# One core: the bias stage and the attention put into one program, with the first splits spread over four steps

## What is computed

```
scores = q @ k.T / 8
x      = log1p(|i - j|) / log1p(max(i, 1))          # 576 x 576
bias   = relu(x * w1 + b1) @ w2                      # 32 hidden, 8 heads
attn   = softmax(scores + bias);   o = attn @ v
h = o @ w_in;   g = s * relu(h)**2 + b;   x1 = g @ w_out
h = x1 @ w2_in; g = h - tanh(h);          out = g @ w2_out
```

## Time and profile before

| | |
|---|---|
| median of 3 runs | 1180.36 us (1180.12 to 1181.59) |
| the profiled execution | 1182.0 us, of which 1180.2 us is the span of the trace |
| PE busy | 1123.6 us (95% of the span) |
| ACT, DVE, POOL busy | 720.2, 629.5, 597.8 us |
| chain that ended last | PE 85% of the span |

### The profile page before, as it was taken

How to read it: one execution, slowest core, us unless ns; L and a number is a source line. 1 busy time by engine, 2 the same in 40 slices (tenths; PEclk the granted TensorE clock), 3 DMA queues, 4 the chain that set the end, 5 groups by cost and what they waited for, 6 DMA issues and landing times.

```text
span 1180.2 us, 17800 instructions
## 1 busy us (share of the span) xinstructions
PE 1123.6 (95%) x6306; PEld 995.0 (84%) x6306; DVE 629.5 (53%) x1090; ACT 720.2 (61%) x1362; POOL 597.8 (51%) x505
## 2 busy tenths in 40 slices
PE   4659878999999999999999999999999999999998
PEld 1138767999999999999999999999988888999998
DVE  5857775744675366447654754566344063260440
ACT  8957785755676477557665765676455264473552
POOL 1014545566465545655655555555455455555553
PEclk9879998999999999999999999999999999999999
DMA  3577773455445544554455454453233333433332
GB/s 127 209 249 200 217 211 93 151 172 178 139 155 159 175 152 142 163 157 141 162 167 171 138 160 156 149 162 125 81 115 107 107 101 105 131 109 124 97 111 75
DMA packets 69657, 172.47 MB, mean 146 GB/s; under 512 B 8704, under 2 KB 15680, under 8 KB 69568
## 3 DMA queue, kind: packets, MB, share of 16 engines
q1 hardware_dynamic: 69280, 171.24, 46.3%
q10 hardware_dynamic: 288, 0.07, 0.0%
HBM read 155.59 MB, written 15.69 MB: 145 GB/s over the span
## 4 chain that ended last, share of the span: by engine, by line
PE 85%; ACT 1%; issue 0%; DVE 0%; ACTq 0%
PE ps_f L652 23%; PE ps_f L654 23%; PE ps_f L653 23%; PE ps_t L477 6%; PE ps_o L442 3%; PE ps_o L444 3%; PE ps_s L464 3%; PE ps_s L465 3%; PE ps_s L458 0%; ACT p_t L499 0%; ACT pth L490 0%; DVE ptl L556 0%; ACT wh L602 0%; DVE xl L628 0%; DVE p_t L544 0%
## 5 line engine op out<-in xcount | busy, mean ns | idle before, releaser
L609 POOL TENSOR_TENSOR wl<-w_raw,wh 128x512 fp32r<-128x512 f32 x320 | 418.3, 1313 | 441.5 <-ACT wh L602 441.3
L652 PE MATMUL ps_f<-xh,wh 128*128 128x464 f32 (+1 forms) x640 | 239.4, 374 | 5.0 <-issue 5.0
L652 PE MATMUL ps_f<-gh,wh 128*128 128x464 f32 (+1 forms) x640 | 238.8, 373 | 0.0
L654 PE MATMUL ps_f<-xh,wl 128*128 128x464 f32 (+1 forms) x640 | 238.5, 373 | 0.0
L653 PE MATMUL ps_f<-xl,wh 128*128 128x464 f32 (+1 forms) x640 | 238.1, 372 | 0.0
L654 PE MATMUL ps_f<-gh,wl 128*128 128x464 f32 (+1 forms) x640 | 237.4, 371 | 0.0
L653 PE MATMUL ps_f<-gl,wh 128*128 128x464 f32 (+1 forms) x640 | 237.3, 371 | 0.0
L602 ACT ACTIVATE wh<-w_raw 128x512 fp32r<-128x512 f32 x320 | 198.0, 623 | 40.0 <-PE ps_f L654 39.8
L544 DVE CUSTOM_DVE_ANT_0 p_t<-ps_s,bias_t 128x576 f32<-128x576 f32 x160 | 120.0, 750 | 94.0 <-PE ps_s L465 93.3
L675 ACT ACTIVATE r_buf<-ps_f 128x464 f32<-128x464 f32 (+1 forms) x160 | 89.2, 557 | 115.0 <-PE ps_f L654 115.0
L490 ACT ACTIVATE pth<-ps_t 128x576 fp32r<-128x576 f32 (+1 forms) x140 | 91.0, 650 | 91.9 <-PE ps_t L477 89.7
(11 more groups left out here) (74 smaller groups left out, 1536.6 us busy)
## 6 DMA issues: line engine op xcount, KB each, us to landing
w_raw<-in_w_in SPq DMA_DIRECT2D x80, 512.0 KB, 3.8
w_raw<-in_w_out SPq DMA_DIRECT2D x80, 512.0 KB, 3.7
bias_t<-bias_flat SPq DMA_DIRECT2D x128, 288.0 KB, 2.9
bias_flat<-stage SPq DMA_DIRECT2D x36, 295.5 KB, 2.1
q_raw<-in_qt SPq DMA_DIRECT2D x32, 288.0 KB, 3.9
k_raw<-in_kt SPq DMA_DIRECT2D x32, 288.0 KB, 4.5
v_raw<-in_vt SPq DMA_DIRECT2D x32, 160.0 KB, 4.1
bias_t<-bias_flat SPq DMA_DIRECT2D x32, 144.0 KB, 4.1
```

The lines of the kernel that those rows point to most:

```text
L609: pool.tensor_tensor(wl[:, b % RING, :, :], w_raw[:, b // 2 % RAW, b % 2, :, :], wh[:, b % RING, :, :].bitcast(F32), ALU.subtract).then_in ...
L652: pe.matmul(acc, hi, rhs_h[:, k0 + kk, 0:T], start=(first and kk == 0), stop=False)
L654: mm = pe.matmul(acc, lo, rhs_h[:, k0 + kk, 0:T], start=False, stop=(last and kk == 3))
```

## The change

- One block in place of two. The four kinds of bias work are functions (`sp_biases`, `act_biases`, `pool_biases`, `dve_biases`, `pe_biases`) which the engines run first; nothing makes the engines meet. SP waits for all stores before the first weight load, because `stage` now lies in the weight buffer `w_raw`, `hid` in `x_raw` (which holds only two, HIDS = 2) and the small tables in `y`.
- The bias network divides by lam at the end: hidden = max(psi * w1 + b1 * lam, 0), where psi * w1 is made once, and the copies multiply by 8 / lam per row (`row_scale`). The constant, the reciprocal of 144 columns and one small matmul go; a reciprocal of 36 columns comes.
- Scores of head 0 go to ps_s and ps_o in turn.
- The splits of unit 0 follow steps (4, 1), (6, 1), (8, 1) and (9, 1). GpSimd's first three low weight parts follow (8, 2), (8, 3) and (8, 4). In `pool_step` the scaling of a pair comes ahead of the k work.
- `FIRST` is 48: steps (9, 1) and (9, 2) move ahead of the first block, which waits for the last low part of these steps; the last two places stay empty.

```diff
-HIDS = 3
+HIDS = 2
+EXTRA = 2
-    FIRST = (H + 1) * NT + 1
+    FIRST = (H + 1) * NT + 1 + EXTRA
...
+        hid, = carve(x_raw, [(HIDS, PACK, S)])
+        stage, psi_t = carve(w_raw, [(RES_BUFS, S + ROW), (S,)])
+        psi_w, lam_c, knee, row_lam, row_inv, row_scale, net_c, w2_s = carve(
+            y, [(S,), (STEPS,), (STEPS,), (PACKS,), (PACKS,), (PACKS,), (2,), (G * H,)])
...
-                        mm = act.activation(hid[:, pack % HIDS, at, 0:n], psi_t[:, 0:n], ACT.Relu,
-                                            scale=slope[:, step:step + 1], bias=b1_c)
+                    mm = act.activation(hid[:, pack % HIDS, at, 0:n], psi_w[:, 0:n], ACT.Relu,
+                                        bias=knee[:, step:step + 1])
...
-                            mm = act.activation(dst, acc[:, 0:hi - lo], ACT.Identity, scale=1.0 / SCALE,
-                                                bias=const[:, 0:1])
+                        mm = act.activation(dst, acc[:, 0:hi - lo], ACT.Copy,
+                                            scale=row_scale[:, pack:pack + 1])
...
-                        mm = dve.tensor_scalar(hid[:, pack % HIDS, at, 0:n], psi_t[:, 0:n],
-                                               slope[:, step:step + 1], nb1_c[:, 0:1], ALU.mult, ALU.max)
+                    mm = dve.tensor_scalar(hid[:, pack % HIDS, at, 0:n], psi_w[:, 0:n],
+                                           knee[:, step:step + 1], 0.0, ALU.add, ALU.max)
...
-                            mm = dve.tensor_scalar(dst[:, ::-1], acc[:, lo - first:hi - first], 1.0 / SCALE,
-                                                   const[:, 0:1], ALU.mult, ALU.add)
+                        mm = dve.tensor_scalar(dst[:, ::-1], acc[:, lo - first:hi - first],
+                                               row_scale[:, pack:pack + 1], None, ALU.mult)
...
+            dve.tensor_scalar(psi_w, psi_t, w1_c, None, ALU.mult).then_inc(table_done, 1)
+            dve.tensor_scalar(knee, lam_c, b1_c, None, ALU.mult).then_inc(table_done, 1)
+            dve.reciprocal(row_inv, row_lam).then_inc(table_done, 1)
+            dve.wait_ge(table_done, 3)
+            dve.tensor_scalar(row_scale, row_inv, 1.0 / SCALE, None, ALU.mult).then_inc(table_done, 1)
...
+        def score_bank(n, t):
+            return ps_o if n == 0 and t % 2 else ps_s
...
-                need(pe, min_done, n * NT + t)
+                if n == 0:
+                    need(pe, min_done, t - 1)
+                    pe.wait_ge(back_done, PACKS - 2 if t == 0 else PACKS)
+                else:
+                    pe.wait_ge(min_done, n * NT + t)
...
         def pool_step(pool, n, t):
+            if t == 0 and n >= 2 and n % 2 == 1:
+                pool_scale(pool, n - 2)
...
-            if t == 0 and n >= 2 and n % 2 == 1:
-                pool_scale(pool, n - 2)
...
         def _(sp):
+            sp_biases(sp)
             load_qk(sp, 1)
+            for i in range(RES_BUFS):
+                sp.wait_ge(stage_stored[i], PACKS // RES_BUFS * DMA)
...
-            for b in range(AHEAD):
-                pool_weights(pool, b)
+                if n == H and 0 <= t - NT + AHEAD:
+                    pool_weights(pool, t - NT + AHEAD)
...
+        SPLIT_FIRST = [(4, 1), (6, 1), (8, 1), (9, 1)]
...
-                if n == H and t == AHEAD:
-                    for kt_ in range(KD - 1):
-                        act_split(act, 0, kt_)
-            act_split(act, 0, KD - 1)
+                if (n, t) in SPLIT_FIRST:
+                    act_split(act, 0, SPLIT_FIRST.index((n, t)))
...
-            pe.wait_ge(pt_lo_done, H * NT)
+            pe.wait_ge(pt_lo_done, H * NT + EXTRA + 1)
```

More of the change, by code:

```diff
@@ L586, in sp_step, with raw_block @@
                 load_v(sp, n + 1)
+        def raw_block(b):
+            half = w_raw[:, b // 2 % RAW, b % 2 * KD * P:(b % 2 + 1) * KD * P]
+            return half.rearrange("p (k n) -> p k n", k=KD)
         def sp_weights(sp, pair):
```

311 lines of the change are left out of this document (145 added, 166 removed).

## The result

The change made the kernel slightly slower: median 1184.57 us (1181.42 to 1189.79, 20 runs) against 1181.66 us (1180.12 to 1182.89, 20 runs), ratio 1.0029, 95% interval 1.0018 to 1.0039. The forecast was 1174.2 us, its range ended at 1178.2, and "slower" had a chance of 0.05. The profiled execution of the changed kernel took 1184.26 us, span 1182.5. The old kernel's runs lie within 2.8 us of each other, the new one's within 8.4, and they go with TensorE's mean granted clock: the five fastest (1181.4 to 1182.3) had 0.990 or 0.991, the two slowest (1188.9 and 1189.8) 0.982 and 0.981. Between kernels this mean says little, since it also counts stretches in which TensorE waits anyway: nine runs of the kernel before, taken beside e13, had 0.980 to 0.987 at 1181.4 to 1183.1 us, in no order.

What follows compares the result with a forecast made beforehand. From 190 us TensorE, always busy, was taken to bound the kernel, so gains had to come ahead of the blocks or remove TensorE work. Gains of 15.75 less losses of 9.6 gave 6.15 us: 1174.2 us, range 1169.5 to 1178.2.

Steps and rivals of the forecast that it cites:

- joint: Between bias stage and head 1: q and k load sooner, head 1 starts earlier; 3.6 us gained, bounds 2.5 and 4.5.
- clock: Ahead of the first block: TensorE idles about 3.2 us and its clock holds at full rate; 2.9 us gained.
- splits: Heads 4, 6 and 8: VectorE waits for ScalarE's rounding and split, then works beside GpSimd; 4.6 us lost.
- start: Start of the bias stage: a reciprocal and a constant leave the path to the first bias work; 0.65 us gained.
- hidden tiles: Bias stage: 72 ScalarE tiles read one per-partition operand less, 0.088 us each; 5.3 us gained after deductions.
- scaling ahead of k: Heads 3, 5 and 7: VectorE's small inverse instruction waits for GpSimd's scaling, 0.57 us each; 1.7 us lost.
- end of the steps alone: From step (9, 0) to the first block: the added steps and last split start the blocks later; 3.3 us lost.
- two steps out of the blocks: Among the blocks: two steps of 1.62 us each leave TensorE's work there; 3.3 us gained.
- two deductions: Taken off the hidden tiles' 6.3 us: VectorE without idle time 0.5 us, TensorE at half clock 0.5 us.
- sign of being wrong: Between bias stage and blocks: the prediction would be wrong if head 1 waited for its bias tiles.
- That the clock falls: Rival, ahead of the blocks: first block runs at half clock, the 2.9 us go, 1177.1 us; chance 0.25.
- "slower" rival: Among the blocks: shifted steps make TensorE wait once a head; 1185.7 us at 0.5 us a head; chance 0.05.

Runs made afterwards that it cites:

- e13: The changed kernel with only the splits' place moved, lower parts of the first three ahead of the output sum in heads 4, 6, 8: 1172.4 us, ratio 0.9924.
- e9: The kernel before with the new bias arithmetic and the first splits spread behind (4,1), (6,1), (8,1), (9,0), nothing else: 1184.2 us, ratio 1.0021.
- e1: The kernel before with the new bias arithmetic alone; its two blocks, order and banks kept: 1174.93 us, ratio 0.9934.
- e4: The changed kernel with the first three weight loads issued behind the steps of heads 3, 4 and 5, not ahead of all steps: 1182.28 us, ratio 1.0005.
- e8: The changed kernel with head 1's q and k loaded behind the store of pack 32, not behind the last bias load: 1183.56 us, ratio 1.0013.
- e12: The changed kernel with splits moved as in e13, scaling behind k work, weights late, q and k early, shorter wait ahead of the blocks: 1165.39 us, ratio 0.9857.
- e14: e12 with the splits back in the old places, three in a row behind (8,3), the fourth behind the last step: 1168.69 us, ratio 0.9888.
- e15: e12 without the two extra steps ahead of the blocks, the fourth split behind (9,0): 1167.62 us, ratio 0.9875.
- e7: The changed kernel with head 0's scores in one pair of banks, as before: 1188.16 us, ratio 1.0042.
- e5: The changed kernel without the two extra steps ahead of the blocks, the fourth split behind (9,0): 1181.12 us, ratio 0.9994.
- e3: The changed kernel with the scaling of a finished pair behind the k work again: 1184.67 us, ratio 1.0019.
- e6: The changed kernel with 20, 8 and 20 unused transposes on TensorE behind steps (8,1), (9,1) and (9,2): 1182.54 us, ratio 1.0006.
- e2: The changed kernel with three splits behind (8,3) and the fourth behind the last step, as before: 1177.01 us, ratio 0.9955.

## Why the prediction was wrong

Three terms failed. The joint, put at +3.6 us, gave nothing, since SP waited 2.1 us longer for the last store and then the bias tiles of head 1 did not land in time; the clock, put at +2.9, fell all the same; and the splits, put at -4.6, cost 6.9 in the profiles and 9 to 12 by the medians of e9 and e13. Another 1.3 us lie in the base: the forecast starts from 1180.36, the median of three runs, and twenty have 1181.66. The terms, each against what the profiles show (before to after, us gained):

| term | predicted | measured | where it is read |
|---|---|---|---|
| start | +0.65 | +0.70 | 6.08 to 5.38 |
| hidden tiles | +5.3 | +6.7 | stage end 72.25 to 64.87, less the start |
| joint | +3.6 | -0.3 (give or take 1) | 7.12 ahead at head 2, less the 7.38 of the stage |
| scaling ahead of k | -1.7 | -2.2 | heads 3, 5 and 7: 0.74 each |
| splits | -4.6 | -6.9 | heads 4 and 6: 2.5 each, head 8: 1.9 |
| end of the steps alone | -3.3 | -3.6 | first block less head 9: 4.82 to 8.43 |
| two steps out of the blocks | +3.3 | +3.3 | first block -5.6, span -2.3 |
| clock | +2.9 | 0 | half clock again in 186 to 192 |
| sum | +6.15 | -2.3 | 1182.0 to 1184.26 |

**Right: start and hidden tiles.** The price of an operand read per partition was 89 ns at 576 columns, 88 were taken. The two deductions, 0.5 us for VectorE and 0.5 for TensorE at half clock, don't show in the sum. By the Trainium skill's 93 ns ("ScalarE: Activation LUTs", What ACT_TABLE_LOAD costs) the term would be 72 x 0.093 = 6.7, close to what was measured. e1 shows that the gain passes through undiminished.

**Wrong: the joint.** The step that failed is that the bias tiles "I expect to land just in time". The scores of head 1 did start at 77.39, forecast 77.5, but by luck: 1.4 us more from the stage made up for 1.3 less from the joint. I had the last bias load follow the stage's end as closely as before, and it came later, since its wait for the last store took 3.9 us in place of 1.8. All thirteen profiled kernels with one block have this wait at 3.9 to 4.9 us, the four with two blocks at 1.8 to 2.1; why is open. Then the first minimum waited for a bias tile until 79.93, 1.2 us after its scores were done, and TensorE, idle for 9.34 us, worked at half clock until past 85 us, as in the earlier trace rows. The prediction had named this wait as a sign of being wrong. The lower bound, 2.5 us, named the cause, the 1.5 MB of weights, and stopped too soon: it priced a late start but not what stood behind it. e4 and e8 each move one load, and head 2 comes 1.6 and 2.3 us earlier than in after, the first within what such kernels scatter there; with both, in e12, e14 and e15, 6.1 to 7.0. e7 leaves open whether the two bank pairs are worth anything: the start of head 1 does not depend on them.

**Mis-sized: the splits.** The mechanism was told rightly, wait for ScalarE and a lower part beside GpSimd, and at heads 4 and 6 the term was 2.2 against 2.5. At head 8, "0.2 more" was 1.9: the hole there was 2.83 us, and TensorE's clock fell to half behind it. e9 and e1 price the spread splits at 9.3 us by themselves, e13 at 12.2 us in the kernel after. Between the profiled executions of e13 and after, 8.9 us apart, 5.0 lie in heads 4 and 6, 3.7 in head 8 and 1.7 ahead of the first block, less 1.0 at head 2 and 1.3 for e13's fall of the clock in head 7. And a hole can cost more than its length: head 4 took 12.95, 12.96 and 13.20 us in after, e5 and e9, where the clock held behind it, and 13.34, 14.20, 14.29, 14.84 and 14.85 in e4, e7, e8, e3 and e6, where it fell. With three such heads an execution this fits the scatter from 1181.4 to 1189.8, in which no run of after with a mean clock of 0.990 or more was over 1182.3; shown it is not, since each kernel has one profile.

**Wrong: the clock.** "I take it that the clock holds" failed. Ahead of the blocks TensorE idled 0.68, 0.95 and then 2.10 us with little work between, and the clock fell at 181.5, already in these small waits. I had counted the last wait alone, and taken 2.8 to 4.1 us as what a clock can stand. In e2 1.38 us, behind 0.67, were enough, and in e9 3.50 us were not. Idle time alone is no rule for when it falls. e6 puts the price of both falls, at head 8 and ahead of the blocks, at 2.0 us by the medians; in the profiles the blocks after the first one's start took 2.6 us less, near the 2.9 of the term.

**Mis-sized a little: scaling and end.** L561 took 0.91 us where 0.73 were taken, 0.74 us a time lost. The Trainium skill ("GPSIMD Engine Reference", Specifications) says that GpSimd's way to SBUF is shared with VectorE; the trace agrees, and what it adds is that the 0.91 us end with GpSimd's instruction (179.11 + 0.91 = 180.02, beside 178.57 + 1.42 = 179.99). The end cost 3.6 for 3.3.

**The rivals.** That the clock falls (0.25) came true, but isn't enough for the result alone. The "slower" rival, waits among the blocks, is refuted: L653 waited 2.1 us in all, ahead of its first block. Slower came by a case that I didn't list: several terms of my own sum, each on the bad side (joint 3.9, clock 2.9, splits 2.3 and scaling 0.5 less), against 1.4 from the tiles. Its parts are not independent, since a delay on VectorE is also a hole for TensorE, behind which the clock can fall; and even their bounds together (joint 1.1, splits 0.9, scaling 0.3, clock 2.9 worse) reach 1179.4 only. The bound that failed most was the joint's, 2.5 where -0.3 came.

**What stays open.** Why a clock falls in one execution and holds in the next at the same idle time isn't settled: it held behind 2.55 and 2.79 us in the profiles of after and e9 at (4, 1) and behind 3.50 in e9's at (8, 1), and fell behind 2.90 in e3's and 1.79 in e4's at (4, 1), and behind 1.38 in e2's. Why SP waits longer for the last store in one block, and whether the second bank pair helps, isn't shown either. Nor is it shown how much of e12's gain over e14 is the clock's.

## What to carry to other kernels

Where two engines hand one tile back and forth, work put between them costs its duration, the wait for the engine that prepares it, and the idle time of the third. Look for a wait that is there already (here 0.9 us once a head, ahead of `o_tmp`) and for the moment when GpSimd is idle: the same four splits cost 12.2 us more in one place than in the other. Where small loads that are needed at once share a queue with large ones that are not, put the large ones behind. And change one part at a time: the arithmetic alone was worth 7.4 us, and the rest of the change took them all.

## What the runs showed of the hardware

- The granted clock fell from 1.00 (2.4 GHz) to 0.50 (1.2 GHz) behind short idle times, and not by their length alone: it fell behind 1.38 us (with 0.67 shortly ahead of it) in e2, where 129 to 133 us had 0.57 with TensorE busy throughout, behind 1.79 in e4 and 2.90 in e3; it held behind 2.79 and 3.50 us in e9.
- VectorE's subtraction of 128x464 from SBUF took 0.64 us beside an idle GpSimd, and 1.07 to 1.90 us beside GpSimd's two-input instructions. A 128x5 instruction of 0.16 us took 0.91 (after), 1.18 (e1) or 1.35 (e2), each time until GpSimd's had ended (e2: 126.25 + 1.35 = 127.60 beside 126.15 + 1.42 = 127.57).
- Transposes that nobody reads kept the clock at 1.00 over the handover of stages in the profiled execution of e6, whose median is 2.0 us under after's.
- SP's wait for the last store of the bias stage took 3.9 to 4.9 us in the thirteen profiled kernels with one block and 1.8 to 2.1 us in the four with two. What makes the difference was not tested.
